# Weights of the next layer prepared piece by piece, another order of two products and of the casts, and later sums of x, in a fused attention and two-layer kernel

## The chip, the cores and the metric

The kernel runs on one core of one Trainium2 chip. The metric is the time of one execution on the device in microseconds (us), as the median of several executions; lower is better. Names of engines: PE is TensorE's matmul, PEld its weight load, DVE is VectorE, ACT is ScalarE, POOL is GpSimd, SP is SyncE, which here only issues DMAs.

## What is computed

```python
scores = scale * (q @ k.T)                       # 4 x 8 heads, 576 x 576, head size 64
keep scores >= rowmax - tau, the rest -1e9
attn = softmax(scores); x = attn @ v             # x: 2304 tokens x 512
h = x @ w_in;  x = (h - tanh(h)) @ w_out         # layer 0, d_ff = 2048
h = x @ w_in2; out = (h * sigmoid(h)) @ w_out2   # layer 1
```

All of it is float32 in and out.

## The kernel before

Every float32 matmul is made of three in a rounded format (fp32r): each operand is split in a high part (a copy by ACT, which rounds) and a low part (the operand less its high part, a subtraction by DVE), and lo·hi, hi·lo and hi·hi are added in PSUM. On top of that each 2 by 2 block product of a layer is done with seven products instead of eight (Strassen's scheme in Winograd's form). They are called m1 to m7 here, their operands include sums of weight blocks (made by POOL, four for each tile of weights, `sums_of`) and sums of blocks of x.

**Stages.** Attention takes the first 304 us. Then come six passes z = 0 to 5: three thirds of the tokens for layer 0 (with tanh), three for layer 1 (with silu). A pass has a hidden stage and a projection.

**The hidden stage** has eight steps j = 0 to 7 (u = 8z + j counts them over all passes). A step runs the seven products of one tile of hidden columns, each six matmuls of 128x384 (`product_of`). PE's order in a step is m1(u), m5(u), m4(u-1), m6(u), m2(u), m3(u), m7(u): m4 belongs to the step before. Around them stand

- ACT: `seed` copies the result of m1 into the bank in which m6 adds; `take_s5` and `take_u2` copy results of m5 and m6 out of PSUM; `nonlinear` applies tanh (or silu) to each of four results "11", "12", "22", "21"; `w_hi_first`, `w_hi_sums` and `w_hi_last` round the next tile of weights in four pieces.
- DVE: `add_u2(u)` and `add_s5(u)` combine results in PSUM; `gate` subtracts tanh in layer 0 (nothing in layer 1); `w_lo(u+1, part)` makes the four low pieces of the next tile of weights.
- POOL: `w_sums_of(u+1)`.
- SP: `load_w(u+2)`, which waits until all four low pieces of tile u are made, since the raw weights have two buffers.

m6(u) waits for `seed(u)`. m4(u-1) waits for `add_s5(u-1)`, which comes behind m7(u-1). m7(u) waits for `take_u2(u)`. `w_hi_first(u+1)` waits for the load of tile u+1 and for m7(u-1).

**The projection** is 28 batches of 12 matmuls; its weights w2 come from a scratch tensor `scr` in HBM through five buffers (`load_w2`), its input from `g_hi_of` (ACT) and `g_lo_of` (DVE), whose first three batches are made in the last steps of the hidden stage.

**Weights of the next layer.** The seven operands of layer 1's output weights are prepared in passes 0 to 3, two tiles of eight in each pass (`NEXT`). The raw tile is loaded into `stage_raw`, POOL makes its four sums, ACT its high parts in three instructions (`next_hi_of`, at steps 1 and 3), DVE its low parts in three instructions (`next_lo_of`, at steps 2 and 4, ahead of gate "11"), and SP writes the 1792 KB to `scr` (`store_next`). The two homes of these tiles share their memory with later tenants: home 1 with the w2 buffers, home 0 with the g_op buffers 1 to 3. So w2 is loaded after home 1 has been stored (`load_w2`), and `g_hi_of` writes buffers 1 to 3 after home 0 has been stored. Five w2 loads are issued together at step 5.

**The end of attention.** POOL normalises each tile of 576 columns (`probs * rinv`), PE transposes it, and on the last tiles follow the last products with v. Between its normalisations POOL makes the four sums of x for pass 0, at the steps in `TAIL_SUMS`; ACT makes the high parts at the steps in `TAIL_HI`; DVE makes the low parts (`x_lo_of`), the first of them ahead of its last two row-sum reciprocals (`rinv`).

All orders are written out by hand: each engine's program is a sequence of calls, and semaphores join them.

Of the kernel before, what the change touches and what calls it, by code (L numbers as in the profile page):

```python
# [13 lines left out]
P = 128  # L14
# [28 lines left out]
L_S = 8  # L43
# [182 lines left out]
def build(nc, q_in, k_in, v_in, tau_in, w_in, scr, out):  # L226
    ctx = ExitStack()
    with ctx:
# [175 lines left out]
        def _(sp):  # L404
# [89 lines left out]
            def load_w2(gb):  # L494
                z, product, q = g_index(gb)
                m = z // SPLITS
                if z < len(NEXT) and gb % BATCHES < W2_SLOTS:
                    sp.wait_ge(next_stored[1], 16 * NEXT_COUNT[NEXT[z][1]])
# [30 lines left out]
            for z in range(PASSES):  # L529
# [3 lines left out]
                for j in range(FP):  # L533
# [3 lines left out]
                    if j >= 2 and j % 2 == 0 and j // 2 <= len(nexts):  # L537
                        store_next(nexts[j // 2 - 1])
                    if j == FP - 3:
                        for i in range(W2_SLOTS):  # L540
                            load_w2(BATCHES * z + i)
# [9 lines left out]
        def _(pool):  # L551
# [5 lines left out]
            def sums_of(raw, sums, done, base):  # L557
# [4 lines left out]
                total(3, raw[:, 3], raw[:, 2], ALU.add)  # L562
                pool.wait_ge(done, base + 1)
                total(4, sums[:, 3, 1], raw[:, 0], ALU.subtract)
                pool.wait_ge(done, base + 2)
                total(5, raw[:, 1], sums[:, 4, 1], ALU.subtract)
                total(6, raw[:, 0], raw[:, 3], ALU.subtract)
# [45 lines left out]
            def next_sums_of(f):  # L613
# [4 lines left out]
                sums_of(stage_raw[u], stage[u][:].bitcast(F32), next_sums, 4 * f)  # L618
# [57 lines left out]
            for z in range(PASSES):  # L676
                nexts = NEXT[z] if z < len(NEXT) else ()
                for j in range(FP):
# [3 lines left out]
                    if j % 2 == 0 and j // 2 < len(nexts):  # L682
                        next_sums_of(nexts[j // 2])

        @block.scalar
        def _(act):
# [104 lines left out]
            def next_hi_of(f):  # L791
                op, raw = stage[NEXT_HOME[f]], stage_raw[NEXT_HOME[f]]
                act.wait_ge(next_sums, 4 * (f + 1))
                act.activation(op[:, 0:3, 0], raw[:, 0:3], ACT.Copy).then_inc(next_hi, 1)
                for s in (slice(3, 5), slice(5, 7)):
                    act.activation(op[:, s, 0], op[:, s, 1].bitcast(F32), ACT.Copy).then_inc(next_hi, 1)
# [132 lines left out]
        def _(dve):  # L929
# [100 lines left out]
            def next_lo_of(f):  # L1030
                op, raw = stage[NEXT_HOME[f]], stage_raw[NEXT_HOME[f]]
# [410 lines left out]
```

## Time and profile before

| | us |
|---|---|
| median of three executions | 1046.44 (1045.47 to 1049.03) |
| the profiled execution, its own time | 1049.05 |
| its span, first to last instruction | 1047.2 |
| PE busy | 1001.8 |
| DVE busy | 827.1 |
| ACT busy | 711.2 |
| POOL busy | 455.2 |

Durations below come from the one profiled execution. Its time is 1.85 us more than its span and 2.61 us above the median. A timeline gives for each instruction, or run of like ones, its start from the beginning of the span, its length, and in brackets how long the engine had been idle before it and what ended that.

### The profile page before, as it was taken

To read this page: it belongs to the slowest core of one execution; us is meant where nothing else is said; L and a number is where in the kernel's file an instruction comes from. 1 tells how busy PE (TensorE), PEld (TensorE's weight loads), DVE (VectorE), ACT (ScalarE), POOL (GpSimd) and SP (SyncE) were. 2 spreads that over 40 slices of the span, in tenths; PEclk is the share of its full clock that TensorE was granted. 3 is DMA by queue.
4 is the path that set the end of the run, shared out by engine and by line. 5 is a ranking of instruction groups with operands and counts; after the bars stand their busy time and mean duration, and the time that the engine had idled before them with its cause. 6 is when DMAs were issued, how large, how long until landed. Compare 5 with 4: busy or idle time off the path is not lost.

```text
span 1047.2 us, 18072 instructions
## 1 busy us (share of the span) xinstructions
PE 1001.8 (96%) x6002; PEld 906.7 (87%) x6002; DVE 827.1 (79%) x1633; ACT 711.2 (68%) x1441; POOL 455.2 (43%) x509
## 2 busy tenths in 40 slices
PE   6999999999998999988999899998899999999998
PEld 5666676667668999987999899988899999999998
DVE  8999999999958799687996889765696549944575
ACT  6999999999956665556646566467573676547543
POOL 5999999999955310353104440063300341013100
PEclk9999999999999999999999999999999999999999
DMA  6245454542224668436673467536585445844286
GB/s 215 93 146 198 158 186 170 180 175 70 107 73 139 232 180 251 131 112 231 208 253 103 157 208 246 193 101 212 184 250 175 128 179 180 252 141 145 86 250 215
DMA packets 57867, 181.00 MB, mean 173 GB/s; under 512 B 5040, under 2 KB 6576, under 8 KB 57776
## 3 DMA queue, kind: packets, MB, share of 16 engines
q1 hardware_dynamic: 57488, 179.78, 51.6%
q8 instruction: 49, 0.80, 0.3%
q14 instruction: 42, 0.34, 0.1%
q10 hardware_dynamic: 288, 0.07, 0.0%
HBM read 145.75 MB, written 34.08 MB: 172 GB/s over the span
## 4 chain that ended last, share of the span: by engine, by line
PE 79%; DMA 8%; POOL 4%; DVE 4%; issue 1%; ACT 0%; SPq 0%; ACTq 0%; DVEq 0%; POOLq 0%
PE b L1370 34%; PE b L1290 20%; PE scores L1251 10%; PE pv L1214 9%; DMA w_raw<-w_in 7%; PE tps L1273 6%; POOL w_sum L560 4%; DVE stage L1034 1%; DVE w_op L1027 1%; DMA scr<-stage 1%; DVE c L1084 0%; POOL stage L560 0%; DVE probs L959 0%; DVE probs L991 0%; POOL probs L634 0%
## 5 line engine op out<-in xcount | busy, mean ns | idle before, releaser
L1290 PE MATMUL b<-x_op,w_op 128*128 128x384 f32 x2016 | 362.6, 339 | 26.4 <-DVE b L1077 16.1
L1290 PEld LDWEIGHTS b<-x_op,w_op 128*128 128x128 f32 x2016 | 353.7, 190 | 33.2 <-issue 19.1
L1370 PE MATMUL b<-g_op,w 128*128 128x384 f32 x2016 | 353.4, 335 | 0.2
L1370 PEld LDWEIGHTS b<-g_op,w 128*128 128x128 f32 x2016 | 350.4, 188 | 2.0 <-DVE c L1084 1.1
L560 POOL TENSOR_TENSOR w_sum<-w_raw 128x256 f32<-128x256 f32 x94 | 79.4, 844 | 294.6 <-DMA w_raw<-w_in 203.1
L1027 DVE TENSOR_TENSOR w_op<-w_raw,w_op 128x512 fp32r<-128x512 f32 x94 | 61.7, 656 | 111.4 <-ACT w_op L779 110.2
L959 DVE TENSOR_SCALAR_CACHE_REDUCE probs<-scores,fine 128x576 f32<-128x576 f32 x144 | 116.8, 811 | 12.1 <-PE scores L1251 11.6
L866 ACT ACTIVATE g_op<-c 128x768 fp32r<-128x768 f32 x96 | 81.3, 847 | 59.4 <-PE b L1370 30.2
L1251 PEld LDWEIGHTS scores<-k_lo,q_parts 128*128 128x128 f32 x336 | 64.0, 193 | 64.9 <-issue 38.5
L634 POOL TENSOR_SCALAR probs<-probs,rinv 128x576 f32<-128x576 f32 x144 | 111.8, 777 | 16.3 <-DVE rinv L984 9.2
L991 DVE SCALAR_TENSOR_TENSOR probs<-scores,stats,probs 128x576 f32<-128x576 f32 x144 | 117.8, 818 | 0.1
L1251 PE MATMUL scores<-k_lo,q_parts 128*128 128x288 f32 x336 | 106.6, 341 | 11.1 <-DVE q_parts L1003 6.0
L739 ACT ACTIVATE probs<-probs,stats 128x576 f32<-128x576 f32 x144 | 111.4, 774 | 4.7 <-DVE probs L991 4.3
L1273 PE MATMUL tps<-ident,probs 128*128 128x128 f32 x656 | 97.5, 276 | 1.7 <-POOL probs L634 1.7
L725 ACT ACTIVATE pT<-tps 128x512 f32<-128x512 f32 x144 | 85.8, 596 | 17.4 <-PE tps L1273 16.4
L560 POOL TENSOR_TENSOR stage<-stage_raw 128x256 f32<-128x256 f32 x16 | 15.2, 952 | 187.5 <-DMA stage_raw<-w_in 187.5
L1115 DVE TENSOR_TENSOR g_op<-c,g_op 128x768 fp32r<-128x768 f32 x96 | 91.9, 957 | 3.1 <-ACT g_op L866 2.6
L1251 PE MATMUL scores<-k_hi,q_parts 128*128 128x288 f32 x336 | 93.1, 300 | 0.0
L1214 PE MATMUL pv<-pT,v_all 128*64 128x288 f32 x512 | 90.6, 436 | 2.7 <-issue 2.6
L1027 DVE TENSOR_TENSOR w_op<-w_sum,w_op 128x512 fp32r<-128x512 f32 x94 | 76.2, 817 | 14.5 <-POOL w_sum L560 12.0
L1273 PEld LDWEIGHTS tps<-ident,probs 128*128 128x128 f32 x656 | 78.6, 141 | 4.7 <-POOL probs L634 2.9
L848 ACT ACTIVATE h_act<-b 128x384 f32<-128x384 f32 x96 | 47.0, 490 | 51.7 <-DVE b L1069 46.4
(89 smaller groups left out, 1321.4 us busy)
## 6 DMA issues: line engine op xcount, KB each, us to landing
w<-scr SPq DMA_DIRECT2D x168, 512.0 KB, 4.5
w_raw<-w_in SPq DMA_DIRECT2D x56, 512.0 KB, 5.2
scr<-w_op SPq DMA_DIRECT2D x8, 1792.0 KB, 8.4
scr<-stage SPq DMA_DIRECT2D x8, 1792.0 KB, 7.0
k_raw<-k_in SPq DMA_DIRECT2D x15, 576.0 KB, 6.1
q_raw<-q_in SPq DMA_DIRECT2D x15, 576.0 KB, 7.0
v_all<-v_in SPq DMA_DIRECT2D x16, 320.0 KB, 3.2
stage_raw<-w_in SPq DMA_DIRECT2D x8, 512.0 KB, 4.4
```

The costliest lines, as they stand in the source:

```text
L560: pool.tensor_tensor(sums[:, slot, 1], a, b, how).then_inc(done, 1)
L634: pool.tensor_scalar(tile, tile, r, 1.0, ALU.mult, ALU.mult).then_inc(norm_done, 1)
L739: act.activation(tile, tile, ACT.Exp, bias=stats[:, c, 0:1], scale=-SCALE / FINE, accum_out=rowsum[:, c:c + 1]).then_inc(exp_done, 1)
L959: dve.tensor_scalar(tile, scores[q % SBUFS][:, :, 0:HALF], fine[:], None, ALU.mult, ALU.max, accum_out=finemax[:, c:c + 1]).then_inc(max_d ...
L991: dve.scalar_tensor_tensor(out=tile, in0=scores[q % SBUFS][:, :, 0:HALF], scalar=stats[:, c, 1:2], in1=tile, op0=ALU.is_lt, op1=ALU.subtra ...
L1027: dve.tensor_tensor(op[:, s, 1], raw[:, s] if part in (0, 3) else sums[:, s, 1], op[:, s, 0].bitcast(F32), ALU.subtract).then_inc(w_split, 1)
L1115: dve.tensor_tensor(g_op[slot][:, 1], source, g_op[slot][:, 0].bitcast(F32), ALU.subtract).then_inc(g_split, 1)
L1214: last = pe.matmul(pv[h * DH:(h + 1) * DH, 0:HALF], v_of(u, c, h), keys[c][h], start=(c == 0), stop=(c == FULL))
L1251: last = pe.matmul(scores[q % SBUFS][:, a, c0:c0 + w], rows, keys, start=(i == 0), stop=(i == len(todo) - 1))
L1273: last = pe.matmul(bank[:, c, :], block, ident[:], is_transpose=True, start=True, stop=True)
L1290: last = pe.matmul(out, a, b, start=fresh and k == 0 and i == 0, stop=k == 1 and i == 2, skip_group_check=True)
L1370: last = pe.matmul(bank[n][kind], x, y, start=fresh and q == 0 and f == 0 and i == 0, stop=q == 3 and f == 1 and i == 2, skip_group_check= ...
```

## The change

It has these parts.

1. The preparation of the next layer's weights is cut into pieces: POOL's sums in two parts at steps 0 to 3 (`NEXT_SUMS_AT`), ACT's high parts one a step at steps 0 to 3 and two at step 4 (`NEXT_HI_AT`; the first of them no longer waits for POOL's sums), DVE's low parts one a step at steps 1 to 4 and two at step 5 (`NEXT_LO_AT`). They stand behind w_lo(u+1, 1) now, ahead of gate "21". The stores go out at steps 4 and 6 (before: 2 and 4). The first tile of a pass now has home 1.
2. PE runs m6(u) ahead of m4(u-1).
3. ACT's and DVE's orders within a step change: `w_hi_first(u+1)` stands ahead of `seed(u)`, `take_u2` ahead of nonlinear "21", `w_hi_last` behind it; w_lo(u+1, 0) stands ahead of the gates "12" and "22", w_lo(u+1, 3) behind gate "11".
4. w2 is loaded in two groups, three at step 5 and two at step 7; in layer 1 a w2 load waits only for the stores of the tiles that it reads. g_hi and g_lo of the first three batches are spread differently.
5. At the end of attention the last two sums of x (for m4 and m7) come behind POOL's last normalisation, their high parts later, and all low parts behind DVE's last reciprocals.
6. `touch` reads weight buffer u instead of buffer 0.

```diff
-NEXT_HOME = {f: i % 2 for fs in NEXT for i, f in enumerate(fs)}
+NEXT_HOME = {f: 1 - i % 2 for fs in NEXT for i, f in enumerate(fs)}
+NEXT_SUMS_AT = {0: (0, 0), 1: (0, 2), 2: (1, 0), 3: (1, 2)}
+NEXT_HI_AT = {0: ((0, 0),), 1: ((0, 1),), 2: ((0, 2),), 3: ((1, 0),), 4: ((1, 1), (1, 2))}
+NEXT_LO_AT = {1: ((0, 0),), 2: ((0, 1),), 3: ((0, 2),), 4: ((1, 0),), 5: ((1, 1), (1, 2))}
+NEXT_STORE_AT = {4: 0, 6: 1}
+W2_AHEAD = {FP - 3: (0, 1, 2), FP - 1: (3, 4)}
+G_AHEAD = {5: 0, 7: 1}
-TAIL_SUMS = {STEPS: (5,), STEPS + 2: (6,), STEPS + 4: (4,), STEPS + 6: (7,)}
-TAIL_HI = (1, 1), (5, 4), (6, 6), (2, 9), (3, 10), (7, 12), (4, 14)
+TAIL_SUMS = {STEPS: (5,), STEPS + 2: (6,), STEPS + L_NORM: (4, 7)}
+TAIL_HI = (1, 1), (5, 4), (6, 6), (2, 9), (3, 10), (7, 15), (4, 18)
```

ACT's order in a pass:

```diff
             def hidden(z):
                 for j in range(FP):
                     u = FP * z + j
+                    if u + 1 < JOBS:
+                        w_hi_first(u + 1)
                     seed(u)
                     if j > 0:
                         nonlinear("22", u - 1)
                     take_s5(u)
                     if u + 1 < JOBS:
-                        w_hi_first(u + 1)
                         w_hi_sums(u + 1, 0)
+                    take_u2(u)
                     if j > 0:
                         nonlinear("21", u - 1)
                     if u + 1 < JOBS:
                         w_hi_sums(u + 1, 1)
-                    take_u2(u)
-                    if u + 1 < JOBS:
                         w_hi_last(u + 1)
                     nonlinear("11", u)
-                    if z < len(NEXT) and j % 2 == 1 and j // 2 < len(NEXT[z]):
-                        next_hi_of(NEXT[z][j // 2])
-                    if j >= FP - 3:
-                        g_hi_of(BATCHES * z + j - FP + 3)
+                    if z < len(NEXT):
+                        for i, part in NEXT_HI_AT.get(j, ()):
+                            next_hi_of(NEXT[z][i], part)
+                    if j in G_AHEAD:
+                        g_hi_of(BATCHES * z + G_AHEAD[j])
                     nonlinear("12", u)
                 nonlinear("22", u)
+                g_hi_of(BATCHES * z + 2)
                 nonlinear("21", u)
```

DVE's order in a pass, and at the end of attention:

```diff
                     if j > 0:
                         add_s5(u - 1)
+                    if u + 1 < JOBS:
+                        w_lo(u + 1, 0)
+                    if j > 0:
                         gate("12", u - 1)
                         gate("22", u - 1)
                     if u + 1 < JOBS:
-                        w_lo(u + 1, 0)
                         w_lo(u + 1, 1)
+                    if z < len(NEXT):
+                        for i, part in NEXT_LO_AT.get(j, ()):
+                            next_lo_of(NEXT[z][i], part)
                     if j > 0:
                         gate("21", u - 1)
                     if u + 1 < JOBS:
                         w_lo(u + 1, 2)
+                    gate("11", u)
+                    if u + 1 < JOBS:
                         w_lo(u + 1, 3)
-                    if z < len(NEXT) and j > 0 and j % 2 == 0 and j // 2 <= len(NEXT[z]):
-                        next_lo_of(NEXT[z][j // 2 - 1])
-                    gate("11", u)
-                    if j >= FP - 2:
-                        g_lo_of(BATCHES * z + j - FP + 2)
+                    if j == FP - 2:
+                        g_lo_of(BATCHES * z)
                     add_u2(u)
                 add_s5(u)
+                g_lo_of(BATCHES * z + 1)
...
             steps(BATCH - 1, range(STEPS, STEPS + L_S), False)
+            steps(BATCH - 1, range(STEPS + L_S, STEPS + L_SUM), False)
             dve.wait_ge(scores_done, SCORED)
-            x_lo_of(0, X_ORDER[0])
-            steps(BATCH - 1, range(STEPS + L_S, STEPS + L_SUM), False)
-            for product in X_ORDER[1:]:
+            for product in X_ORDER:
                 x_lo_of(0, product)
```

PE's order in a step:

```diff
                     m1_m5(u)
+                    m6(u)
                     if u > FP * z:
                         m4(u - 1)
-                    m6_m2_m3_m7(u)
+                    m2_m3_m7(u)
```

The order of the instructions shows it at three places. In all of them b11_0 to b22_0 are the result banks of an even step, b11_1 to b22_1 those of an odd one. The first is PE in pass 0, step 2: before, and then with the change.

```order
L1290 MATMUL b11_0<-x_op,w_op0 128x384 x6
L1290 MATMUL b12_0<-x_op,w_op0 128x384 x6
L1290 MATMUL b21_1<-x_op,w_op1 128x384 x6
L1290 MATMUL b21_0<-x_op,w_op0 128x384 x6
L1290 MATMUL b11_0<-x_op,w_op0 128x384 x6
L1290 MATMUL b12_0<-x_op,w_op0 128x384 x6
L1290 MATMUL b21_0<-x_op,w_op0 128x384 x6
```

```order
L1311 MATMUL b11_0<-x_op,w_op0 128x384 x6
L1311 MATMUL b12_0<-x_op,w_op0 128x384 x6
L1311 MATMUL b21_0<-x_op,w_op0 128x384 x6
L1311 MATMUL b21_1<-x_op,w_op1 128x384 x6
L1311 MATMUL b11_0<-x_op,w_op0 128x384 x6
L1311 MATMUL b12_0<-x_op,w_op0 128x384 x6
L1311 MATMUL b21_0<-x_op,w_op0 128x384 x6
```

The third and fourth rows have changed places: m6 of this step (b21_0) now runs ahead of m4 of the step before (b21_1).

The second is ACT in the same step, from nonlinear "12" of step 1 (h_act1<-b12_1) on: before, and then with the change.

```order
L848 ACTIVATE h_act1<-b12_1 128x384
L824 ACTIVATE b21_0<-b11_0 128x384
L848 ACTIVATE h_act0<-b22_1 128x384
L832 ACTIVATE s5_0<-b12_0 128x384
L779 ACTIVATE w_op1<-w_raw1 128x2x256
L784 ACTIVATE w_op1<-w_sum1 128x2x256
L848 ACTIVATE h_act1<-b21_1 128x384
L784 ACTIVATE w_op1<-w_sum1 128x2x256
L838 ACTIVATE u2_0<-b21_0 128x384
L789 ACTIVATE w_op1<-w_raw1 128x256
L848 ACTIVATE h_act0<-b11_0 128x384
L848 ACTIVATE h_act1<-b12_0 128x384
```

```order
L862 ACTIVATE h_act1<-b12_1 128x384
L788 ACTIVATE w_op1<-w_raw1 128x2x256
L838 ACTIVATE b21_0<-b11_0 128x384
L862 ACTIVATE h_act0<-b22_1 128x384
L846 ACTIVATE s5_0<-b12_0 128x384
L793 ACTIVATE w_op1<-w_sum1 128x2x256
L852 ACTIVATE u2_0<-b21_0 128x384
L862 ACTIVATE h_act1<-b21_1 128x384
L793 ACTIVATE w_op1<-w_sum1 128x2x256
L798 ACTIVATE w_op1<-w_raw1 128x256
L862 ACTIVATE h_act0<-b11_0 128x384
L809 ACTIVATE stage1<-stage1 128x2x256
```

The rounding of the raw weights (w_op1<-w_raw1 128x2x256) now stands between nonlinear "12" and the seed (b21_0<-b11_0), and u2 is taken ahead of nonlinear "21". A single rounding of a stage piece follows nonlinear "11".

The third is DVE around the low parts of the next layer's weights, pass 0, step 2, from add_s5(1) on: before, and then with the change.

```order
L1077 TENSOR_TENSOR b22_1<-b21_1,s5_1 128x384
L1084 TENSOR_TENSOR c12<-b12_1,h_act1 128x384
L1084 TENSOR_TENSOR xT<-b22_1,h_act0 128x384
L1027 TENSOR_TENSOR w_op1<-w_raw1,w_op1 128x2x256
L1027 TENSOR_TENSOR w_op1<-w_sum1,w_op1 128x2x256
L1084 TENSOR_TENSOR c21<-b21_1,h_act1 128x384
L1027 TENSOR_TENSOR w_op1<-w_sum1,w_op1 128x2x256
L1027 TENSOR_TENSOR w_op1<-w_raw1,w_op1 128x256
L1034 TENSOR_TENSOR stage0<-stage_raw0,stage0 128x3x256
L1034 TENSOR_TENSOR stage0<-stage0 128x2x256 x2
L1084 TENSOR_TENSOR c11<-b11_0,h_act0 128x384
L1069 TENSOR_TENSOR b12_0<-b12_0,u2_0 128x384
```

```order
L1094 TENSOR_TENSOR b22_1<-b21_1,s5_1 128x384
L1043 TENSOR_TENSOR w_op1<-w_raw1,w_op1 128x2x256
L1101 TENSOR_TENSOR c12<-b12_1,h_act1 128x384
L1101 TENSOR_TENSOR xT<-b22_1,h_act0 128x384
L1043 TENSOR_TENSOR w_op1<-w_sum1,w_op1 128x2x256
L1051 TENSOR_TENSOR stage1<-stage1 128x2x256
L1101 TENSOR_TENSOR c21<-b21_1,h_act1 128x384
L1043 TENSOR_TENSOR w_op1<-w_sum1,w_op1 128x2x256
L1101 TENSOR_TENSOR c11<-b11_0,h_act0 128x384
L1043 TENSOR_TENSOR w_op1<-w_raw1,w_op1 128x256
L1086 TENSOR_TENSOR b12_0<-b12_0,u2_0 128x384
```

Before, three subtractions of the stage stood together ahead of gate "11" and add_u2 (the row stage0<-stage0 counts two); now one stands there a step, and the last low piece of the weights comes behind gate "11".

## Rows read from the trace of the kernel before

**Rows 1.** The page: busy time by engine; DMA issues with size and us to landing.

```profile
PE 1001.8 (96%) x6002; PEld 906.7 (87%) x6002; DVE 827.1 (79%) x1633; ACT 711.2 (68%) x1441; POOL 455.2 (43%) x509
...
w_raw<-w_in SPq DMA_DIRECT2D x56, 512.0 KB, 5.2
```

**Rows 2.** Stretches, hidden stages of passes 0 to 4: length, PE PEld DVE ACT POOL busy, clock.

```profile
304.50:369.10 64.60, 60.17 (x333) 58.41 (x332) 51.02 (x83) 43.60 (x95) 30.80 (x36) 0.97 0.52 180
428.76:496.92 68.16, 60.24 (x331) 58.36 (x331) 53.69 (x83) 44.12 (x96) 31.66 (x36) 0.97 0.49 170
556.59:621.34 64.75, 59.98 (x331) 58.31 (x330) 51.53 (x83) 44.04 (x96) 31.38 (x36) 0.97 0.52 179
681.04:748.42 67.38, 59.57 (x331) 57.71 (x331) 39.53 (x55) 45.85 (x97) 31.31 (x36) 0.99 0.50 172
808.57:866.87 58.30, 57.48 (x332) 57.16 (x332) 29.48 (x49) 41.68 (x91) 20.82 (x28) 1.00 0.42 145
```

**Rows 3.** Timeline of PE: start, us, line, tiles [idle before, releaser].

```profile
455.47 16.49 PE L1290 MATMUL b<-x_op,w_op 128*128 128x384 f32 x84 [3.50 <-DVE b L1077]
...
495.55 1.32 PE L1290 MATMUL b<-x_op,w_op 128*128 128x384 f32 x6 [2.20 <-ACT u L838]
...
822.03 44.99 PE L1290 MATMUL b<-x_op,w_op 128*128 128x384 f32 x258 [0.82 <-ACT u L838]
```

**Rows 4.** Timeline of DVE in pass 1, steps 2 and 3.

```profile
447.00 1.22 DVE L1027 TENSOR_TENSOR w_op<-w_sum,w_op 128x512 fp32r<-128x512 f32 x1
...
449.29 0.96 DVE L1027 TENSOR_TENSOR w_op<-w_raw,w_op 128x256 fp32r<-128x256 f32 x1
450.17 1.49 DVE L1034 TENSOR_TENSOR stage<-stage_raw,stage 128x768 fp32r<-128x768 f32 x1
451.58 2.34 DVE L1034 TENSOR_TENSOR stage<-stage 128x512 fp32r<-128x512 f32 x2
...
454.31 0.55 DVE L1069 TENSOR_TENSOR b<-b,u 128x384 f32<-128x384 f32 x1
454.78 0.55 DVE L1077 TENSOR_TENSOR b<-b,s 128x384 f32<-128x384 f32 x1
...
457.71 0.69 DVE L1027 TENSOR_TENSOR w_op<-w_sum,w_op 128x512 fp32r<-128x512 f32 x1
```

**Rows 5.** Timeline of POOL in pass 1.

```profile
447.75 1.06 POOL L560 TENSOR_TENSOR stage<-stage_raw,stage 128x256 f32<-128x256 f32 x1
...
463.95 0.73 POOL L560 TENSOR_TENSOR w_sum<-w_raw 128x256 f32<-128x256 f32 x1 [9.45 <-DMA w_raw<-w_in]
```

**Rows 6.** Timeline of ACT in pass 1.

```profile
454.90 0.49 ACT L848 ACTIVATE h_act<-b 128x384 f32<-128x384 f32 x1 [6.55 <-DVE b L1069]
...
456.43 0.64 ACT L779 ACTIVATE w_op<-w_raw 128x512 fp32r<-128x512 f32 x1
```

**Rows 7.** Timeline of SP's queue in pass 1: start, us, DMA issued.

```profile
453.95 0.38 SPq L491 DMA_DIRECT2D scr<-stage  x1
454.42 5.87 SPq L474 DMA_DIRECT2D w_raw<-w_in  x2
```

**Rows 8.** Timeline of POOL in pass 4: its first sums of weights.

```profile
817.42 0.74 POOL L560 TENSOR_TENSOR w_sum<-w_raw 128x256 f32<-128x256 f32 x1 [64.99 <-DMA w_raw<-w_in]
```

**Rows 9.** Timeline of POOL at the end of attention.

```profile
285.72 1.85 POOL L602 TENSOR_TENSOR x_sum<-xT 128x768 f32<-128x768 f32 x1
...
289.30 0.75 POOL L634 TENSOR_SCALAR probs<-probs,rinv 128x576 f32<-128x576 f32 x1 [1.01 <-DVE rinv L984]
291.31 4.53 POOL L634 TENSOR_SCALAR probs<-probs,rinv 128x576 f32<-128x576 f32 x2 [1.27 <-DVE rinv L984]
```

**Rows 10.** Timeline of DVE at the end of attention.

```profile
289.80 1.05 DVE L1061 TENSOR_TENSOR x_op<-xT,x_op 128x768 fp32r<-128x768 f32 x1
...
291.28 1.83 DVE L1057 TENSOR_TENSOR x_op<-x_sum,x_op 128x768 fp32r<-128x768 f32 x2
```

**Rows 11.** Timeline of PE at the end of attention.

```profile
295.89 0.75 PE L1273 MATMUL tps<-ident,probs 128*128 128x128 f32 x4 [1.11 <-POOL probs L634]
```

More of the change, by code:

```diff
@@ L506, in load_w2 @@
                     else:
-                        sp.wait_ge(next_stored[u], 16 * sum(home == u for home in NEXT_HOME.values()))
+                        sp.wait_ge(next_stored[u], 16 * sum(NEXT_HOME[f] == u for f in range(2 * q + 2)))
                 sp.dma_start(w2[gb % W2_SLOTS][:].bitcast(F32).rearrange("p f a c -> p (f a c)"),
@@ L536, in _ @@
                         load_w(u)
[L537 to L540, printed above, removed]
+                    if j in NEXT_STORE_AT and nexts:
+                        store_next(nexts[NEXT_STORE_AT[j]])
+                    if j in W2_AHEAD:
+                        for i in W2_AHEAD[j]:
                             load_w2(BATCHES * z + i)
@@ L555, in _, with sums_of @@
                                pattern=[[-1, P]], channel_multiplier=1).then_inc(consts_ready, 1)
-            def sums_of(raw, sums, done, base):
+            def sums_of(raw, sums, done, base, wanted=(0, 2)):
                 def total(slot, a, b, how):
                     pool.tensor_tensor(sums[:, slot, 1], a, b, how).then_inc(done, 1)
[L562 to L567, printed above, removed]
+                if 0 in wanted:
+                    total(3, raw[:, 3], raw[:, 2], ALU.add)
+                    pool.wait_ge(done, base + 1)
+                    total(4, sums[:, 3, 1], raw[:, 0], ALU.subtract)
+                if 2 in wanted:
+                    pool.wait_ge(done, base + 2)
+                    total(5, raw[:, 1], sums[:, 4, 1], ALU.subtract)
+                    total(6, raw[:, 0], raw[:, 3], ALU.subtract)
             def stage_piece(f, piece):
@@ L611, in w_sums_of, with next_sums_of @@
                 sums_of(w_raw[u % 2], w_sum[u % 2], w_sums, 4 * (u - 1))
-            def next_sums_of(f):
+            def next_sums_of(f, part):
                 u = NEXT_HOME[f]
@@ L617, in next_sums_of @@
                     pool.wait_ge(next_stored[u], 16 * (NEXT_COUNT[f] - 1))
-                sums_of(stage_raw[u], stage[u][:].bitcast(F32), next_sums, 4 * f)
+                sums_of(stage_raw[u], stage[u][:].bitcast(F32), next_sums, 4 * f, (part,))
             def steps(B, ks, first):
@@ L681, in _ @@
                         w_sums_of(u)
-                    if j % 2 == 0 and j // 2 < len(nexts):
-                        next_sums_of(nexts[j // 2])
+                    if j in NEXT_SUMS_AT and nexts:
+                        i, part = NEXT_SUMS_AT[j]
+                        next_sums_of(nexts[i], part)
         @block.scalar
@@ L789, in w_hi_last, with next_hi_of @@
                 act.activation(w_op[u % 2][:, 2, 0], w_raw[u % 2][:, 2], ACT.Copy).then_inc(w_hi, 1)
[L791 to L796, printed above, removed]
+            def next_hi_of(f, part):
+                u = NEXT_HOME[f]
+                s, op, raw = (slice(0, 3), slice(3, 5), slice(5, 7))[part], stage[u], stage_raw[u]
+                if part == 0:
+                    act.wait_ge(next_loaded[u], 16 * NEXT_COUNT[f])
+                    if f in NEXT_BEFORE:
+                        act.wait_ge(next_stored[u], 16 * (NEXT_COUNT[f] - 1))
+                else:
+                    act.wait_ge(next_sums, 4 * f + 2 * part)
+                act.activation(op[:, s, 0], raw[:, s] if part == 0 else op[:, s, 1].bitcast(F32),
+                               ACT.Copy).then_inc(next_hi, 1)
             def x_hi_of(z, product):
@@ L1028, in w_lo, with next_lo_of @@
                                   op[:, s, 0].bitcast(F32), ALU.subtract).then_inc(w_split, 1)
[L1030 to L1035 removed]
+            def next_lo_of(f, part):
+                s, op, raw = (slice(0, 3), slice(3, 5), slice(5, 7))[part], stage[NEXT_HOME[f]], stage_raw[NEXT_HOME[f]]
+                dve.wait_ge(next_hi, 3 * f + part + 1)
+                if part == 1:
+                    dve.wait_ge(next_sums, 4 * f + 3)
+                dve.tensor_tensor(op[:, s, 1], raw[:, s] if part == 0 else op[:, s, 1].bitcast(F32),
+                                  op[:, s, 0].bitcast(F32), ALU.subtract).then_inc(next_lo, 1)
             def x_sum_of(z, product):
```

11 lines of the change are left out of this document (4 added, 7 removed).

## The prediction

> **What bounds the kernel now.** The page comes first [rows 1]: PE is busy for 96% of the span, no other engine for more than 79%. So what a faster kernel can win here is idle PE time, and slow matmuls behind it. The stretches tell where that is [rows 2]. A hidden stage is 330 matmuls and in pass 4 takes 58.30 us, with PE busy for 57.48; pass 5 repeats it to 0.01 us. With the same matmuls the stages of passes 0 to 3 take 64.60, 68.16, 64.75 and 67.38. Against 57.48 in each, the six lose 7.1 + 10.7 + 7.3 + 9.9 + 0.8 + 0.8 = 36.6 us. That is the most that changes of order in these stages can give. The granted clock, 0.97 in passes 0 to 2 and 1.00 in pass 4, is part of it. The projections run without a gap and are left out.
>
> The timeline of PE names the stalls [rows 3]. At 455.47 PE had been idle for 3.50 us behind DVE's add_s5 (L1077): that is m4 of the step before. At 495.55 it had waited 2.20 us for take_u2 (L838), and at 822.03, in pass 4, 0.82 us for the same. The timelines of DVE and ACT give the cause of the first [rows 4, 6]. In step 2 DVE runs the three stage pieces together, 1.49 + 2.34 us, from 450.17 to 453.9. Only then come add_u2 at 454.31 and add_s5 at 454.78, and ACT had stood idle for 6.55 us. The same block comes again in step 4. The wait for u2 in step 7 comes from the loads: SP issues the 1792 KB store at 453.95 and the next weights behind it at 454.42 [rows 7]; POOL gets these only at 463.95 [rows 5], 9.5 us later, and all casts of the next weights, which stand ahead of take_u2, are late.
>
> **The scale of a step.** 258 matmuls in 44.99 us [rows 3] are 0.174 each, so a product is 1.04 us and a step of seven is 7.3. I count from the start of m1. In the new order m6 is due at 2.1, m4 at 3.1, m7 at 6.2.
>
> **Stages in pieces, m4 behind m6 (passes 0 to 2).** No work is added or removed; six instructions of DVE, six of ACT and eight of POOL per pass move. The block of 3.8 us is gone. add_s5 may now come 1.04 us later than before without holding m4. I take all of the m4 and u2 stalls away, and ask what is late next. It is the seed. ACT runs nonlinear "12", the first weight cast and the seed one after another, about 0.4 + 0.52 + 0.49 (lengths of 0.49, 0.64 and 0.49, overlapping by 0.1 at each change) [rows 6]; the seed has the shape of nonlinear "12". Hence the seed is done 1.45 after DVE's add_u2 of the step before, and m6 waits when add_u2 ends later than 0.6 into the step. Before, the cast was behind the seed and m6 was due at 3.1, so this path had 1.6 us more.
>
> How late is add_u2? DVE's period from one add_u2 to the next is: six operations on PSUM at 0.47 (starts of 454.31 and 454.78 [rows 4]) = 2.8; 0.6 of waiting for the first cast; and the pieces that read only SBUF. Those depend on POOL. The cast remainder of 128x512 took 0.69 at 457.71, when POOL stood idle, and 1.22 at 447.00, when POOL was making stage sums [rows 4, 5]. I take 1.0 + 1.15 for the first two low pieces, 1.25 for the stage piece, 0.65 + 0.35 for the last two, since POOL works for about 5.4 us in steps 0 to 3 and its work comes early in the step. Sum 2.8 + 0.6 + 4.4 = 7.8, which is 0.5 over PE's 7.3. Steps 1 to 3 give 1.5, less about 0.3 of slack at the start; the two pieces of step 5 and g_lo of step 6 add 0.9. That leaves 2.1 us of stalls in a pass. The bounds: with 0.69 for every piece the period is below 7.3 and nothing is left; with the longest row for each (1.22, 1.22, 1.49, 0.69, 0.96) it is 9.0, so 1.7 in each of three steps, and with the later steps about 7 a pass. I take the lower half because POOL is idle for half of each step in passes 0 to 2 (31 of 65 us busy) [rows 2]. So 3 x 2.1 = 6.3 stays of 25.1.
>
> **Pass 3** has no gates, so DVE has room (39.5 us busy) [rows 2]. There and in passes 4 and 5 the first step counts. The weights for step 2 are loaded at the start of the pass; in pass 4 POOL gets them at 817.42 [rows 8], 2.6 us after m1 of step 1 began at 814.8 (one step of six products after 808.57). The cast now blocks the seed until then: 817.42 + 0.52 + 0.47 + 0.05 = 818.46, while m6 is due at 816.9. That costs 1.6 us in passes 4 and 5, where the old order ran the seed ahead of the cast and lost 0.8. In pass 4 the output of pass 3 is stored ahead of this load; in pass 3 two loads of 512 KB stand there instead, about a third less, so I take half, 0.8. In passes 0 to 2, where nothing is stored either and the pass began with the same two loads, the old order showed no wait in step 1; I take 0.1 in all. Left: 6.3 + 0.1 + 0.8 + 3.2 = 10.4 of 36.6. **The stages give 26.2 us.**
>
> **DMA order.** The stores leave at steps 4 and 6, each behind a load of weights and a full step ahead of the next. A store and one load of weights together take about 9.5 us [rows 5, 7], so the load behind it meets its tail, not all of it. A load issued at 7.1 of a step (behind gate "11") must land by 1.0 of the second step after, 8.5 us later; in the row it took 9.5 directly behind a store [rows 5, 7]. I cost it at nothing; its cover is those 8.5 us. The split w2 loads are costed at nothing too: batch 3 is needed 7 us after the last step ends. `touch` changes no length.
>
> **End of attention.** DVE's first x_lo (1.05) [rows 10] stood ahead of the last reciprocals, and POOL waited 1.27 for them [rows 9]. Then the last two normalisations took 4.53 for two, against 0.75 alone, beside DVE's run of subtractions [rows 9, 10]. PE stood idle for 1.11 before the last transposes at 295.89 [rows 11]. Now the first of the two can run ahead of DVE's run, and only the last is slowed: it ends about 2.3 earlier, of which PE can use 1.9. Against it, both sums of 1.85 [rows 9] come behind it and hold ACT's cast for m7 until about 299, close to the copy of the first result with v; I take 0.4 for that. **1.5 us**, between 0 and 2.5.
>
> The Trainium skill, "SBUF — State Buffer", section "Who interferes with whom", says that VectorE and GpSimd share one port pair under an exclusive lock held for a whole instruction. The 4.53 us for two agree. By this rule every SBUF subtraction that meets a sum of POOL waits it out, and the sum would be that of rival B, whose terms come from the long rows alone.
>
> **Sum.** 26.2 + 1.5 = 27.7. From the profiled 1049.05 that is 1021.3; from the median 1046.44 it is **1018.7, say 1019**.
>
> **Rivals.**
> - B, DVE becomes the bound. The period is 9.0 in steps 1 to 3 and pieces of step 5 are long too: 7 us a pass stay instead of 2.1, so 15 more: 1034 at the worst, 1029 with part of it. For it: 1.49 and 0.96 were measured with POOL busy [rows 4]. Against: these rows lie in a stretch in which POOL ran for 12 us on end; now it stops each step.
> - C, loads behind stores. If two loads a pass land 9.5 after issue, the cast starts at 2.0, the seed ends at 3.2, m6 waits 1.1: 2 x 4 x 1.1 = 9, so 1028.
> - D, slower. The same mechanism in all steps: cast ahead of seed, loads issued behind gate "11". It costs nothing while loads land within 8.5 us and decides when all take 9.4: 1.0 in each of 41 steps is 41, less the 10 already counted 31, which is 3 above the 27.7 gained. With all at 9.5 it is 45 less 10: 1054, and PE waits for the seed in every step. Against it: the median load of weights lands 5.2 us after its issue [rows 1].
> - E, the change does not do what it says: the same DVE work (51 to 54 us in a stage) [rows 2] only moves, and each m4 stall comes back as a seed stall of like size. 1045.
>
> **How the numbers follow.** Forecast 0.68, B 0.12, C 0.12, D 0.03, E 0.05. About 0.3% (3 us) is what a measurement can tell from no change. Faster: 0.68 + 0.12 + 0.12 + 0.01 of E = 0.93; same 0.04; slower 0.03. The forecast's own range is 1011 (all stage pieces short, the full gain at the end) to 1026. The range of 8 in 10 takes in C and the nearer part of B: 1010 to 1030.
>
> **What would show it.** The hidden stages of passes 0 to 3 last 58 to 61 us; passes 4 and 5 about 59; no wait of m4 for L1094's add_s5 over 1 us; some waits of m6 for the seed (L838) of 0.3 to 1.6. Stages still near 65 would make it wrong, as would waits for the seed in most steps, or stages of passes 4 and 5 over 61.

## The result and the profile after

The changed kernel takes 1016.48 us in the median (1016.26 to 1018.34, four executions), beside 1047.14 us (1045.47 to 1049.03, four executions too) for the kernel before: a ratio of 0.970 with a 95% interval of 0.968 to 0.972, some 31 us less. The forecast was 1019 us. The span of the profiled execution fell from 1047.2 to 1014.5 us, by 32.7.

The page's head of the changed kernel answers to [rows 1]:

```profile
span 1014.5 us, 18094 instructions
## 1 busy us (share of the span) xinstructions
PE 991.1 (98%) x6002; PEld 900.0 (89%) x6002; DVE 830.2 (82%) x1633; ACT 715.9 (71%) x1441; POOL 462.4 (46%) x509
```

DVE, ACT and POOL are busy for about as long as before (3 to 7 us more). What went is PE's idle time, 22.0 us of it, and 10.7 us of its busy time, since fewer matmuls are slow.

The stretches of the six hidden stages, with columns as in [rows 2]: start and end, length, busy time of PE, PEld, DVE, ACT and POOL, granted clock, DMA share and rate.

```profile
301.13:360.20 59.07, 58.30 (x332) 57.27 (x332) 52.02 (x85) 43.79 (x94) 33.37 (x37) 1.00 0.57 197
419.90:479.62 59.72, 58.26 (x331) 57.02 (x331) 50.14 (x83) 44.16 (x95) 31.30 (x36) 1.00 0.57 194
539.33:597.62 58.29, 57.96 (x332) 57.04 (x331) 49.73 (x83) 44.24 (x95) 32.29 (x36) 1.00 0.57 199
657.31:714.95 57.64, 57.62 (x332) 57.16 (x332) 39.07 (x54) 46.24 (x97) 31.79 (x36) 1.00 0.59 202
774.48:833.34 58.86, 57.56 (x332) 57.10 (x331) 30.57 (x48) 41.75 (x90) 22.79 (x28) 1.00 0.41 144
892.87:951.68 58.81, 57.56 (x332) 57.14 (x331) 28.29 (x44) 40.20 (x86) 19.52 (x24) 1.00 0.36 126
```

They sum to 352.39 us against 381.49 before: 29.1 of the 32.7 us. Passes 0 to 3 gained 5.5, 8.4, 6.5 and 9.7 us; passes 4 and 5 lost 0.6 and 0.5. The granted clock is 1.00 in all six, where it was 0.97 in three of them. The first stage starts at 301.1 instead of 304.5, another 3.4 us, and that makes 32.5.

What PE still waits for from the end of attention on (who waited for whom: us in total, times, longest):

```profile
PE b L1311 <- ACT b L838: 5.0, 8, 1.3
PE pv L1235 <- issue: 1.0, 1, 1.0
PE b L1393 <- DVE g_op L1132: 0.5, 3, 0.2
```

The same view of the kernel before had these two rows:

```profile
PE b L1290 <- DVE b L1077: 16.1, 6, 3.5
PE b L1290 <- ACT u L838: 10.0, 8, 2.4
```

The 16.1 us of m4 behind add_s5 and the 10.0 us of m7 behind u2 are gone. In their place stand eight waits of m6 for the seed (L838). The timeline shows the longest in layer 0 link by link, at step 2 of pass 1, which began at 433.95. DVE, ACT and PE:

```profile
435.21 0.55 DVE L1086 TENSOR_TENSOR b<-b,u 128x384 f32<-128x384 f32 x1
```

```profile
435.79 0.49 ACT L862 ACTIVATE h_act<-b 128x384 f32<-128x384 f32 x1 [2.54 <-DVE b L1086]
436.18 0.62 ACT L788 ACTIVATE w_op<-w_raw 128x512 fp32r<-128x512 f32 x1
436.70 0.48 ACT L838 ACTIVATE b<-b 128x384 f32<-128x384 f32 x1
```

```profile
437.23 36.80 PE L1311 MATMUL b<-x_op,w_op 128*128 128x384 f32 x210 [1.04 <-ACT b L838]
```

add_u2 ends at 435.76, tanh, the weight cast and the seed follow, and m6 starts 1.47 us after add_u2's end. The forecast had 1.45 for this chain. ACT had stood idle for 2.54 us before it, so the question is why add_u2 was late. One step earlier POOL and ACT (L788, idle for 0.60 us) had waited for the load of the weights:

```profile
427.60 0.73 POOL L566 TENSOR_TENSOR w_sum<-w_raw 128x256 f32<-128x256 f32 x1 [1.93 <-DMA w_raw<-w_in]
```

What that load costs is measured below, under "The load for step 2 first".

### The profile page after: what moved, and what is told of

Its sections match the earlier page's. It is cut to its first block, busy times and chain, and to the rows that moved or that the text cites. A ratio compares the mean times of both kernels' runs of the same rounds, so it can differ in the third digit from the quotient of the medians.

```text
span 1014.5 us, 18094 instructions
## 1 busy us (share of the span) xinstructions
PE 991.1 (98%) x6002; PEld 900.0 (89%) x6002; DVE 830.2 (82%) x1633; ACT 715.9 (71%) x1441; POOL 462.4 (46%) x509
## 4 chain that ended last, share of the span: by engine, by line
PE 86%; DVE 5%; DMA 3%; issue 2%; ACT 1%; POOL 1%; SPq 0%; ACTq 0%; DVEq 0%; POOLq 0%
PE b L1393 31%; PE b L1311 28%; PE scores L1272 10%; PE pv L1235 10%; PE tps L1294 7%; DMA w_raw<-w_in 3%; DVE g_op L1132 1%; DVE w_op L1043 1%; DVE x_sum L1066 1%; DVE c L1118 1%; POOL w_sum L566 1%; DVE c L1101 0%; DVE b L1086 0%; ACT b L838 0%; DVE stage L1051 0%
## 5 line engine op out<-in xcount | busy, mean ns | idle before, releaser
L1311 PE MATMUL b<-x_op,w_op 128*128 128x384 f32 x2016 | 355.4, 335 | 5.1 <-ACT b L838 5.0
L1311 PEld LDWEIGHTS b<-x_op,w_op 128*128 128x128 f32 x2016 | 349.0, 188 | 9.7 <-ACT b L838 8.6
L566 POOL TENSOR_TENSOR w_sum<-w_raw 128x256 f32<-128x256 f32 x94 | 75.2, 800 | 260.5 <-DMA w_raw<-w_in 132.1
L642 POOL TENSOR_SCALAR probs<-probs,rinv 128x576 f32<-128x576 f32 x144 | 109.3, 759 | 19.5 <-DVE rinv L1000 12.7
L566 POOL TENSOR_TENSOR stage<-stage_raw 128x256 f32<-128x256 f32 x16 | 18.8, 1173 | 179.4 <-DMA stage_raw<-w_in 179.4
L880 ACT ACTIVATE g_op<-g_sum 128x768 fp32r<-128x768 f32 x48 | 40.7, 848 | 59.9 <-DVE g_sum L1118 59.9
```

What stands on the lines that cost most here:

```text
L566: pool.tensor_tensor(sums[:, slot, 1], a, b, how).then_inc(done, 1)
L642: pool.tensor_scalar(tile, tile, r, 1.0, ALU.mult, ALU.mult).then_inc(norm_done, 1)
L880: act.activation(g_op[gb % G_SLOTS][:, 0], source, ACT.Copy).then_inc(g_hi, 1)
L1311: last = pe.matmul(out, a, b, start=fresh and k == 0 and i == 0, stop=k == 1 and i == 2, skip_group_check=True)
```

## The experiments

In each of the three sets the kernel before ran on the same chip, with medians of 1048.4, 1049.3 and 1048.2 us. Ratios to it are the measure between sets; the changed kernel has 0.970 in both of its measurements, the one above and one in the third set.

### The block of three stage pieces back

```diff
-NEXT_LO_AT = {1: ((0, 0),), 2: ((0, 1),), 3: ((0, 2),), 4: ((1, 0),), 5: ((1, 1), (1, 2))}
+NEXT_LO_AT = {3: ((0, 0), (0, 1), (0, 2)), 5: ((1, 0), (1, 1), (1, 2))}
```

> The changed kernel, with DVE's six low pieces of the next weights bunched again, three at step 3 and three at step 5; all else as changed. Theory (the gain of the stages comes from cutting DVE's block of 3.8 us): the block comes back, about 2.5 to 3.8 us, add_u2 is that much later, the seed with it, and m6 waits some 2 to 3 us in steps 4 and 6 of passes 0 to 3: 8 x 2.5 = 20, so 1030 to 1037. Rival (the gain comes from m4 behind m6, which gives add_s5 1.04 us more, and from the order of the casts): at most 1 us in each pass comes back, 1017 to 1021.

Measured: 1031.65 us, ratio 0.984 (0.983 to 0.985), about 15 us slower than the changed kernel. The six stages take 367.1 us in place of 352.4; 9.4 us of the difference are idle time and 5.3 are busy time of PE, at a granted clock of 0.97 in passes 0 to 2. PE's waits for the seed rose from 5.0 to 14.5 us:

```profile
PE b L1311 <- ACT b L838: 14.5, 13, 2.2
```

In the timeline of DVE the block stands in step 3 of pass 0, and the m6 of step 4 waits behind it:

```profile
326.35 1.49 DVE L1051 TENSOR_TENSOR stage<-stage_raw,stage 128x768 fp32r<-128x768 f32 x1
327.76 1.83 DVE L1051 TENSOR_TENSOR stage<-stage 128x512 fp32r<-128x512 f32 x2
```

```profile
333.87 16.45 PE L1311 MATMUL b<-x_op,w_op 128*128 128x384 f32 x84 [2.18 <-ACT b L838]
```

The block costs its time on PE with m4 behind m6 and the new casts as well, so the rival falls. But it gives back only 14.7 of the 29.1 us that the stages had gained. The waits for u2 stay away with the block back in DVE's order, so the other half has another cause.

### m6 first, alone

The kernel before, with only this edit:

```diff
                     m1_m5(u)
+                    m6(u)
                     if u > FP * z:
                         m4(u - 1)
-                    m6_m2_m3_m7(u)
+                    m2_m3_m7(u)
```

> The kernel before with m6(u) ahead of m4(u-1) on PE and nothing else. Theory: m6 needs the seed, which ACT can give only behind nonlinear 12, that is behind the same block on DVE: m6 is due at 2.1 us into step 3 and waits until about 6.0, where m4 waited until 5.7. No gain, or a loss of 0.3 us at each of seven or so stalls: 1046 to 1051 beside a kernel before at about 1048. Rival (add_s5's 1.04 us more is worth something by itself): the 16.1 us of waits of m4 shrink by 1 us each: 1042 or less.

Measured: 1050.67 us, ratio 1.001 (0.9997 to 1.002). It gives nothing. The waits changed their name and grew a little:

```profile
PE b L1290 <- ACT b L824: 19.6, 8, 3.3
PE b L1290 <- ACT u L838: 7.4, 8, 2.6
```

The same block of DVE ends in the seed (L824) now instead of in add_s5, 19.6 for 16.1 us; the waits for u2 shrank from 10.0 to 7.4. Together 27.0 for 26.1.

### m4 first again, in the changed kernel

```diff
                     m1_m5(u)
-                    m6(u)
                     if u > FP * z:
                         m4(u - 1)
+                    m6(u)
                     m2_m3_m7(u)
```

> The changed kernel with PE's old order, m4(u-1) ahead of m6(u). Theory: with the pieces cut add_s5 ends by 1.5 us into the step and m4 is due at 2.1, so m4 does not wait; the seed is due at 3.1 instead of 2.1, so the waits of m6 for the seed (5.0 us in all, 1.30 and 1.25 of them in passes 4 and 5) mostly vanish: 1013 to 1016, no slower than the changed kernel. Rival: m4 behind m6 carries a good part of the gain: waits of m4 for add_s5 come back, 1 us or more in four steps of each of passes 0 to 3, 1021 or more.

Measured: 1011.16 us, ratio 0.964 (0.963 to 0.966): over 5 us faster than the changed kernel, the intervals apart, and below the range that was expected. Its waits:

```profile
PE b L1311 <- DVE b L1094: 1.8, 4, 0.7
PE pv L1235 <- issue: 1.0, 1, 1.0
PE b L1393 <- DVE g_op L1132: 0.6, 3, 0.2
PE b L1311 <- ACT b L838: 0.4, 2, 0.2
```

Eight waits of 5.0 us for the seed became two of 0.4, and m4 waits 1.8 us in all. So m4 behind m6, part 2 of the change, is a loss once the pieces are cut: add_s5 is nearly early enough without it, and it takes 1.04 us from the seed, which is not. By the lengths of the six stages the gain is 352.4 less 347.6, 4.8 us: 2.9 of idle time and 1.8 of PE's busy time. A part of the 1.8 is that the first matmul after a wait is longer: in the changed kernel the one at 437.23 took 443 ns, against a median of 334. The rest of it has not been traced.

### The old order of the casts

ACT and DVE as before within a step (first cast behind `take_s5`, `take_u2` behind the third cast, first low piece behind two gates, last ahead of gate "11"), once with the changed PE order, once with m4 first. ACT's part (DVE's is the change's own piece, reversed):

```diff
-                    if u + 1 < JOBS:
-                        w_hi_first(u + 1)
                     seed(u)
                     if j > 0:
                         nonlinear("22", u - 1)
                     take_s5(u)
                     if u + 1 < JOBS:
+                        w_hi_first(u + 1)
                         w_hi_sums(u + 1, 0)
-                    take_u2(u)
                     if j > 0:
                         nonlinear("21", u - 1)
                     if u + 1 < JOBS:
                         w_hi_sums(u + 1, 1)
+                    take_u2(u)
+                    if u + 1 < JOBS:
                         w_hi_last(u + 1)
```

> The changed kernel with ACT's and DVE's old order within a step (first cast behind take_s5, take_u2 behind nonlinear 21 and the third cast; first low piece behind the gates, last ahead of gate 11), pieces and PE's order kept. Theory: the seed no longer waits for the cast, so the 1.30 and 1.25 us in passes 4 and 5 turn into waits of m7 for u2 of about 0.8, and the seed waits in passes 0 to 2 go: 1014 to 1017. Rival (the casts' order carries part of the gain): waits of m7 for u2 in several steps of passes 0 to 3, 1020 or more.

> The changed kernel with both PE's old order and the old order of ACT and DVE within a step: of the change to the stages only the pieces (with their stores, homes and the split w2 loads) are left. Theory (the pieces carry the gain): the waits for the seed go, m7's waits for u2 of 0.8 us in passes 4 and 5 stay: 1011 to 1013, and so as fast as the run with PE's old order alone (1011.16). Rival (once m4 is first, the new order of the casts is needed): 1015 or more, with waits of m4 for add_s5 or of m7 for u2 in most steps with stage pieces.

Measured: 1016.01 us, 0.969 (0.9675 to 0.970), with m6 first; 1013.07 us, 0.966 (0.964 to 0.9675), with m4 first. With m6 first the waits for u2 of 0.8 us came in passes 4 and 5, as expected, but the seed's waits of layer 0 did not go:

```profile
PE b L1309 <- ACT b L838: 3.6, 4, 1.3
PE b L1309 <- ACT u L852: 1.6, 2, 0.8
```

These four stand in step 2 of passes 0 to 3 (1.13, 1.31, 0.30 and 0.85 us). The cast is not ahead of the seed in this kernel, so it cannot be their cause. With m4 first:

```profile
PE b L1309 <- DVE b L1094: 1.7, 2, 1.0
PE b L1309 <- ACT u L852: 1.6, 2, 0.8
```

The order of the casts is worth nothing that can be told with m6 first (its waits are 3.6 + 1.6 us in place of 5.0), and perhaps 1.5 us with m4 first, where the intervals still touch. The last kernel has nothing of the changes within a step but the pieces, and it is faster than the changed kernel: the pieces, with their stores, homes, w2 loads and g_hi and g_lo, are the whole gain of the stages. How that gain divides among them was not tested beyond the first experiment: DVE's block is about half, and the other half may lie in the pieces of ACT and POOL, in the later stores or in the split w2 loads.

### The load for step 2 first

```diff
+                load_w(FP * z + 2)
+                if z > SPLITS:
+                    store(z - 1)
                 for f in nexts:
                     load_next(z, f)
                 for j in range(FP):
                     u = FP * z + j + 2
-                    if u < JOBS:
+                    if j > 0 and u < JOBS:
                         load_w(u)
...
-                elif z >= SPLITS:
-                    store(z)
```

> The changed kernel with the load of the weights for step 2 of each pass issued first, ahead of the store of the last pass's output and of the stage loads. Theory: it lands before step 1, so the seed waits of 1.30 and 1.25 us in passes 4 and 5 and the 1.04 and 0.15 of pass 1 go: 1016.5 less about 3.5 gives 1013. Rival (the seed waits there come from DVE or POOL and not from the load): 1016 or more.

> The last one together with PE's old order, everything else as changed. Theory: of the waits left with PE's old order (0.69 in pass 1, 0.73 in pass 3, 0.22 and 0.21 in passes 4 and 5, all in step 1 or 2) most go with the load: 1011.2 less about 2 gives 1009 to 1010. Rival: nothing is left to gain there, 1011 or more.

Measured: 1011.16 us, 0.964 (0.9625 to 0.966), and with m4 first as well 1008.23 us, 0.961 (0.960 to 0.963). The waits for the seed with the load alone moved, beside 5.0 us in eight:

```profile
PE b L1312 <- ACT b L839: 0.8, 3, 0.3
```

The first thing POOL does in pass 4 shows why. In the changed kernel, then with the load first:

```profile
783.32 0.72 POOL L566 TENSOR_TENSOR w_sum<-w_raw 128x256 f32<-128x256 f32 x1 [63.80 <-DMA w_raw<-w_in]
```

```profile
779.25 0.74 POOL L567 TENSOR_TENSOR w_sum<-w_raw 128x256 f32<-128x256 f32 x1 [61.56 <-PE b L1312]
```

POOL no longer waits for the DMA but for PE's m7 (`w_sums_of` asks for it). SP's queue, the same two kernels in the same order, shows what moved:

```profile
776.06 13.15 SPq L480 DMA_DIRECT2D w_raw<-w_in  x3
```

```profile
762.85 0.38 SPq L480 DMA_DIRECT2D w_raw<-w_in  x1
```

The load lands 7.2 us after its issue in the first and 6.6 us in the second. So it is not much faster on its way; it is issued 13 us earlier. SP issues in order, `store` waits for the last results of the pass and `load_next` for the last batch of the projection, and whatever stands behind them waits too. In pass 1 the issue moves from 421.59 to 409.80 in the same way.

The gain is 5.3 us between the medians and 5.6 us by the stages (352.4 less 346.8), more than the 3.5 expected. Every seed wait outside step 7 went with it, those of steps 1 and 2 in passes 0 and 1 too, so they had begun with the late load, not with DVE's load of work. With m4 first nothing is left: five of the stages are one unbroken row, here that of pass 1, and pass 0 is broken only by its two first matmuls:

```profile
418.56 57.47 PE L1312 MATMUL b<-x_op,w_op 128*128 128x384 f32 x330
```

### The end of attention

All of it undone, then each half:

```diff
-TAIL_SUMS = {STEPS: (5,), STEPS + 2: (6,), STEPS + L_NORM: (4, 7)}
-TAIL_HI = (1, 1), (5, 4), (6, 6), (2, 9), (3, 10), (7, 15), (4, 18)
+TAIL_SUMS = {STEPS: (5,), STEPS + 2: (6,), STEPS + 4: (4,), STEPS + 6: (7,)}
+TAIL_HI = (1, 1), (5, 4), (6, 6), (2, 9), (3, 10), (7, 12), (4, 14)
```

```diff
-            steps(BATCH - 1, range(STEPS + L_S, STEPS + L_SUM), False)
             dve.wait_ge(scores_done, SCORED)
-            for product in X_ORDER:
+            x_lo_of(0, X_ORDER[0])
+            steps(BATCH - 1, range(STEPS + L_S, STEPS + L_SUM), False)
+            for product in X_ORDER[1:]:
                 x_lo_of(0, product)
```

> The changed kernel with the old end of attention: sums of x for m4 and m7 between the normalisations, first low part ahead of the last two reciprocals. In the changed kernel the first stage starts 3.4 us earlier than before. Theory: all of that is this part, so 1019.5 to 1020.2, first stage from 304.4. Rival: part of the 3.4 us is scatter between executions and the part is worth the predicted 1.5: 1018.

> The changed kernel with only the sums of x and their casts put back between the normalisations; DVE's low parts stay behind its last reciprocals. Theory (the 1.4 to 1.7 us of the end of attention come from DVE's order: the last reciprocal no longer waits for a low part of 1.05 us and the last but one normalisation is no longer beside DVE's run): as fast as the changed kernel or up to 0.6 faster, since ACT's cast for m7 no longer stands before the copy of the result with v (1.02 us wait of PE there): 1.0 lower to equal. Rival (the sums' place carries it): 1 to 1.7 us slower.

> The changed kernel with only DVE's first low part put back ahead of its last two reciprocals; the sums stay behind the last normalisation. Theory (DVE's order carries it): slower by 1 to 1.7 us, first stage from 302.3 or later. Rival (the sums' place carries it): equal to the changed kernel within 0.5.

> The changed kernel itself once more, on the same chip as the next three, to compare them with it: a ratio of 0.970 to the kernel before. Both theories of the others expect this.

Measured: both halves undone 1018.78 us, 0.972 (0.970 to 0.974); only the sums back 1016.07, 0.969 (0.968 to 0.971); only DVE's order back 1017.26, 0.971 (0.969 to 0.972); the changed kernel in the same set 1016.97, 0.970 (0.969 to 0.972). By the ratios the whole part is worth 1.8 us, with intervals that touch. The starts of the first stage in the traces are finer: 302.3 with both undone, 300.9 in the changed kernel, 300.4 with the sums back, 301.0 with DVE's order back. So it is worth 1.4 us, and either half alone has it. One trace of each kernel scatters more than that suggests: six more with the changed end start the stage between 300.9 and 301.5. Counted from the last product with v ahead of the last transposes (`pv<-pR`, at 292.05 with both undone, 292.15 in the changed kernel), which leaves out what lies earlier, the four are 10.23, 8.70, 8.23 and 8.68 us, so the part is worth 1.5. The theory that DVE's order carries it falls, and so does its rival. The last normalisations of POOL, with both undone, in the changed kernel, and with DVE's order back:

```profile
290.92 4.53 POOL L642 TENSOR_SCALAR probs<-probs,rinv 128x576 f32<-128x576 f32 x2 [1.27 <-DVE rinv L1000]
```

```profile
291.23 2.07 POOL L642 TENSOR_SCALAR probs<-probs,rinv 128x576 f32<-128x576 f32 x1 [0.43 <-DVE rinv L1000]
```

```profile
291.19 2.26 POOL L642 TENSOR_SCALAR probs<-probs,rinv 128x576 f32<-128x576 f32 x2 [1.27 <-DVE rinv L1000]
```

In the third case POOL still waits 1.27 us for the reciprocal, but then needs 2.26 for two instead of 4.53. The timelines of DVE and POOL there show what spared it:

```profile
291.15 0.96 DVE L1074 TENSOR_TENSOR x_op<-x_sum,x_op 128x768 fp32r<-128x768 f32 x1
295.34 2.49 DVE L1074 TENSOR_TENSOR x_op<-x_sum,x_op 128x768 fp32r<-128x768 f32 x1 [3.23 <-POOL x_sum L610]
```

```profile
295.20 1.81 POOL L610 TENSOR_TENSOR x_sum<-xT 128x768 f32<-128x768 f32 x1
```

With the sums late, DVE's second summed low part waits for POOL's third sum, as `x_lo_of` asks, and its run of subtractions stops while POOL normalises. With both undone DVE's run has no such stop: four subtractions follow one another from 290.89 to 294.92. The subtraction at 295.34 began 0.14 us behind a sum of POOL and took 2.49 us; the one at 291.15 began 0.04 us ahead of POOL's normalisations and took 0.96.

The rest of the 3.4 us is not the change's. In these two stretches, from 293 us to the first stage, of the kernel before and of the kernel with the old end, POOL's rows are the same, but not the granted clock (the column before the last two):

```profile
293.00:305.00 12.00, 9.73 (x59) 5.54 (x58) 4.38 (x5) 5.20 (x11) 6.27 (x6) 0.86 0.01 1
```

```profile
293.00:302.50 9.50, 7.53 (x54) 4.51 (x55) 4.45 (x4) 4.50 (x10) 5.88 (x6) 1.00 0.01 2
```

A clock of 0.86 over 12 us means, as an estimate, that for 3.4 us PE ran at the lower of its two levels, 1.2 instead of 2.4 GHz, after idling for 0.60 and 1.11 us. The kernel with the old end idled for the same 0.60 and 1.11 us and kept 2.4 GHz. So did the kernel before with m6 first alone, whose attention is that of the kernel before; its row for the same 12 us:

```profile
293.00:305.00 12.00, 9.74 (x68) 6.50 (x67) 4.93 (x5) 5.81 (x13) 6.38 (x6) 1.00 0.07 10
```

Its POOL rows and idle times are the same to 0.02 us, and its first stage starts at 302.8 instead of 304.2. So the drop is scatter between executions. From the end of the last normalisation to the first stage the kernel before took 8.4 us and the one with the old end 6.8, so the drop cost 1.5 us of the profiled execution of before; the remaining 0.4 to 0.5 us of the 3.4 lie earlier, where the traces already stand that far apart.

### What the experiments point to

m4 first, the load first, and ACT's cast of x for m7 behind the copy of the first result with v:

```diff
-TAIL_HI = (1, 1), (5, 4), (6, 6), (2, 9), (3, 10), (7, 15), (4, 18)
+TAIL_HI = (1, 1), (5, 4), (6, 6), (2, 9), (3, 10), (7, 17), (4, 18)
```

> PE's old order, loads first, and ACT's cast of x for m7 behind the copy of the first result with v instead of ahead of it. Theory: the copy no longer waits for POOL's last sum, PE's wait there falls from 1.03 to the 0.56 of the kernel before: 1007.8, a ratio of 0.961 or a little less. Rival: the cast is then late for m7 of the first step, or the wait stays: 1008.2 or more.

Measured: 1007.76 us (1007.67 to 1008.10), ratio 0.962 (0.960 to 0.963), about 9 us below the changed kernel and by the median the fastest of all; by the ratio it can't be told from the one without this last edit. PE's wait before the second half of the products with v fell as expected, to the 0.56 us that the kernel before had:

```profile
298.11 2.16 PE L1236 MATMUL pv<-pT,v_all 128*64 128x288 f32 x16 [0.56 <-issue]
```

## Why the prediction was right, point by point

- **What bounds the kernel, and the cause of the stalls**: right. The stages gave 29.1 us of the 36.6 that were named as the most, and the block of three pieces, put back, cost 15 us in a kernel that differed in nothing else. For the waits for u2, which the text laid to loads behind stores, no run isolates the cause; they stayed away when the block came back.
- **Stages in pieces**: the sum left 6.3 us of stalls in passes 0 to 2 for DVE's pace and 0.1 for the load at their start; their lengths now exceed 3 x 57.48 by 4.6. The total is near, but that is in part luck, because the two terms are mis-sized in opposite ways. With the load first the excess is 2.3 us (58.21 + 58.25 + 58.28 less 172.44), so the load had about 2.3 where 0.1 was taken, and for DVE's pace at most 2.3 is left where 6.3 was taken. The chain of seed behind cast behind tanh behind add_u2 is the one named (1.47 for 1.45), but DVE's period is not 7.8 in each of steps 1 to 3. In the changed kernel the first of them in pass 1 is 9.33 (add_u2 at 425.88, then at 435.21), behind the late load, and the next 7.05. With the load first they are 7.86, 7.18 and 7.45, a mean of 7.50:

```profile
425.58 0.55 DVE L1087 TENSOR_TENSOR b<-b,u 128x384 f32<-128x384 f32 x1
433.44 0.55 DVE L1087 TENSOR_TENSOR b<-b,u 128x384 f32<-128x384 f32 x1
440.62 0.55 DVE L1087 TENSOR_TENSOR b<-b,u 128x384 f32<-128x384 f32 x1
448.07 0.55 DVE L1087 TENSOR_TENSOR b<-b,u 128x384 f32<-128x384 f32 x1
```

- **m4 behind m6**: the text gave it 1.04 us of room for add_s5 and, in the same paragraph, 1.6 us less for the seed, and never set one against the other. That is the step that failed. The runs show that the room was hardly needed and the seed's was: 5 us given away, and still 2.9 (1011.16 less 1008.23) with the load first.
- **Pass 3 and passes 4 and 5**: 0.8 was forecast to be left in pass 3, 0.2 is. In passes 4 and 5 3.2 were forecast and 2.7 are left, by waits of 1.30 and 1.25 us for the seed. The cause, the load behind the store of the output, was shown by moving it. What it cost was the wait of the store on SP's queue more than the transfer of the store.
- **DMA order at nothing**: held for the stores at steps 4 and 6. They land 8.0 to 9.3 us after issue, the median load of weights now 3.8 us (5.2 in [rows 1]), and no PE wait in steps 5 to 7 exceeds 0.3 us. It did not hold for the order at the start of a pass, which cost 5.6 us in all, where 4.1 were taken in the two points on the passes.
- **End of attention**: 1.5 us forecast, 1.5 by the traces counted from `pv<-pR`. The mechanism was half told: that the late sums would stop DVE's run was not seen, and the cast for m7 cost 0.46 us (1.02 for 0.56), where 0.4 was taken.
- **Sum**: 27.7 forecast, 30.7 between the medians. The stages gave 2.9 more than forecast (29.1 for 26.2), which is the difference. The profiled spans differ by 2.0 more than the medians, and the clock drop of 1.5 us in the one profiled execution of before explains most of that.
- **Rivals**: B, with the long rows in every step, is out: one period of add_u2 was 9.3 us, behind the late load, and the stages of layer 0 lost 4.6 in all. C, D and E are out by the same lengths, though a late load did hold the seed as in C, at the start of a pass. The Trainium skill ("SBUF — State Buffer", "Who interferes with whom") says that VectorE with two SBUF inputs and GpSimd reading SBUF lock each other out for a whole instruction. Single rows agree: POOL's sum at 295.20 ends 1.67 us after DVE's subtraction at 295.34 began, and the subtraction took 2.49, near the 2.63 of waiting that out and then running for 0.96. The time of rival B, which the prediction drew from that rule, did not come.

## What to carry to other kernels

When background work is late for the critical engine, ask first how it is bunched: one instruction of DVE a step in place of three in a row gave half of the stages' gain here, with the same work. When one consumer is moved behind another to give its input more time, the other one's input loses that time; set both due times beside both ready times before moving anything. And put the load that is due first ahead of the stores and loads on its queue that have to wait for something: here it was the wait, not the transfer, that made it late.

## What was not expected of the hardware

- The granted clock in the same stretch, after the same two idle times of 0.60 and 1.11 us, was 0.86 in one profiled execution and 1.00 in two others. The lower level (0.50 from 296.5 to 297.8 us) came right behind the idle 1.11 us in the one, and not at all in the others.
- A subtraction of DVE that began behind a sum of POOL took 2.49 us, against 0.96 for one that began ahead of POOL, and two normalisations of POOL beside DVE's run 4.53 against 0.75 for one. A late dependency that keeps the two apart (2.26 for the two) helped as much as the order that was meant to.
